# Products with v of the half-density slots placed behind the first share of the next slot

## What is computed

```python
scores = where(causal, -1e9, q @ k.T / 8 + min(-(cum[i] - cum[j]), 0))   # 4 batches x 8 heads, 576 positions, head size 64
x = softmax(scores) @ v                                                  # 2304 tokens x 512
h = maximum(maximum(x @ w1, x @ w2), x @ w3)                             # 512 -> 768
y = h @ w_out                                                            # 768 -> 512
out = ((y @ w_a) * (y @ w_b)) @ w_out2                                   # 512 -> 1536 -> 512
```

## Time and profile before

| | us |
|---|---|
| median of three runs | 954.92 |
| the profiled execution | 955.04 |
| its span, first to last instruction | 953.3 |
| TensorE matmul busy | 912.0 (96%) |
| VectorE busy | 641.0 (67%) |
| ScalarE busy | 482.3 (51%) |
| GpSimd busy | 339.1 (36%) |

### The profile page before, as it was taken

The page is one execution under the profiler, slowest core; times in us unless marked ns, Lnnn a source line. Parts: engine busy times, 40 slices in busy tenths (PEclk is TensorE's granted clock), DMA queues, the critical chain, the costliest instruction groups (busy, mean ns, idle before and its releaser), DMA issues.

```text
span 953.3 us, 16860 instructions
## 1 busy us (share of the span) xinstructions
PE 912.0 (96%) x5992; PEld 895.2 (94%) x5992; DVE 641.0 (67%) x1369; ACT 482.3 (51%) x1071; POOL 339.1 (36%) x453
## 2 busy tenths in 40 slices
PE   3779899999999999999999999999999999999998
PEld 2578899999999999999999999999999999999998
DVE  6889878877766667664226587868577675676750
ACT  4777776676565655644223445443344443444420
POOL 6867555544243342331001423342133422234200
PEclk9999999999999999999999999999999999999999
DMA  3645232222222122200030342222131112111101
GB/s 117 217 154 159 76 110 66 66 67 93 66 63 59 41 88 66 63 9 15 15 122 2 117 138 95 88 68 73 39 134 60 51 50 76 53 58 54 45 1 67
DMA packets 32225, 71.42 MB, mean 75 GB/s; under 512 B 3600, under 2 KB 18032, under 8 KB 32112
## 3 DMA queue, kind: packets, MB, share of 16 engines
q1 hardware_dynamic: 32144, 70.36, 23.3%
HBM read 60.40 MB, written 9.88 MB: 74 GB/s over the span
## 4 chain that ended last, share of the span: by engine, by line
PE 93%; issue 2%; DVE 2%; ACT 1%; POOL 1%; DMA 1%; SPq 0%; POOLq 0%; DVEq 0%; ACTq 0%
PE bank L1417 28%; PE bank L1292 24%; PE bank L1424 16%; PE bank L1312 8%; PE bank L1243 6%; PE bank L1273 6%; PE bank L1259 5%; DVE soft L942 0%; POOL soft L548 0%; DMA qk_st<-cum_row 0%; DMA qk_raw<-in_qk 0%; ACT soft L619 0%; ACT qk_st L610 0%; DMA x_raw<-in_s 0%; POOL qk_st L539 0%
## 5 line engine op out<-in xcount | busy, mean ns | idle before, releaser
L548 POOL TENSOR_SCALAR soft<-soft,rden 128x576 f32<-128x576 f32 (+4 forms) x160 | 102.3, 658 | 215.5 <-DVE rden L928 215.5
L1292 PE MATMUL bank<-xs_hi,w_hi 128*128 128x256 f32 (+1 forms) x576 | 173.7, 302 | 2.5 <-DVE xs_lo L963 1.9
L1292 PE MATMUL bank<-xs_hi,w_lo 128*128 128x256 f32 (+1 forms) x576 | 170.4, 296 | 0.0
L1292 PE MATMUL bank<-xs_lo,w_hi 128*128 128x256 f32 (+1 forms) x576 | 170.3, 296 | 0.0
L942 DVE CUSTOM_DVE_ANT_0 soft<-bank,causal 64x576 f32<-64x576 f32 (+4 forms) x160 | 85.3, 540 | 46.1 <-PE bank L1243 44.7
L619 ACT ACTIVATE soft<-soft,neg_max 64x576 f32<-64x576 f32 (+4 forms) x160 | 96.0, 600 | 36.0 <-DVE neg_max L942 34.8
L1292 PEld LDWEIGHTS bank<-xs_hi,w_hi 128*128 128x128 f32 x576 | 109.1, 189 | 4.0 <-DVE xs_lo L963 2.1
L1292 PEld LDWEIGHTS bank<-xs_lo,w_hi 128*128 128x128 f32 x576 | 109.3, 190 | 1.1
L1292 PEld LDWEIGHTS bank<-xs_hi,w_lo 128*128 128x128 f32 x576 | 109.1, 189 | 0.0
L1243 PE MATMUL bank<-qk_st 128*128 128x256 f32 (+4 forms) x384 | 92.8, 358 | 16.9 <-DMA qk_st<-cum_row 14.0
L951 DVE TENSOR_TENSOR pt_lo<-bank,pt_hi 128x320 fp32r<-128x320 f32 (+4 forms) x160 | 76.0, 488 | 47.3 <-ACT pt_hi L626 45.3
(11 more groups left out here) (127 smaller groups left out, 2188.8 us busy)
## 6 DMA issues: line engine op xcount, KB each, us to landing
qk_raw<-in_qk SPq DMA_DIRECT2D x32, 576.0 KB, 3.9
raw_even<-in_w SPq DMA_DIRECT2D x18, 512.0 KB, 3.6
raw_odd<-in_w SPq DMA_DIRECT2D x17, 512.0 KB, 3.4
w_raw<-in_w SPq DMA_DIRECT2D x16, 384.0 KB, 3.9
v_raw<-in_v SPq DMA_DIRECT2D x32, 160.0 KB, 2.2
y_raw<-y_dram SPq DMA_DIRECT2D x3, 1536.0 KB, 8.3
outT<-o_stage SPq DMA_DIRECT2D x24, 192.0 KB, 1.9
qk_raw<-in_qk SPq DMA_DIRECT2D x8, 256.0 KB, 3.2
```

The lines of the kernel that those rows point to most:

```text
L548: nc.gpsimd.tensor_scalar(part, part, rden[n % 2][:, i:i + 1], 1.0, ALU.mult, ALU.mult).then_inc(prob_done, 1)
L1292: ins = nc.tensor.matmul(up_ps[g][:, 0:width1(c)], up1_w(w, f, g, kc), x[:, kc, 0:width1(c)], start=(kc == 0 and at == 0), stop=(kc == KC ...
```

## The change

The product of job n - 2 moves from the end of slot n - 1 to slot n, behind its first share, for the slots n = 10 to 24. In slot 24 the product of job 23 keeps its place at the end as well, since slot 25 is of the other kind. ScalarE's `other_half` and VectorE's `x_add` of the moved products move too: behind the exponentials of tiles 0 and 1, and behind `h_lo_sub`. All waits stay as they are.

```diff
--- before.py
+++ after.py
@@ -135,6 +135,12 @@
 def sparse(n):
 
     return place(n)[0] is not None and place(n)[0] < DENSE
+
+
+def outputs_of(n):
+
+    after = n - 2 if sparse(n - 1) else None
+    return after, None if sparse(n + 1) else n - 1
 
 
 def tile_count(n):
@@ -691,9 +697,12 @@
                 rows, downs, rest, ahead = rows_of(n), downs_of(n), rest_of(n), ahead_of(n)
                 if pending_row(n) is not None:
                     h_hi_copy(*pending_row(n))
-                other_half(m - 1)
+                if outputs_of(n)[0] is None:
+                    other_half(m - 1)
                 exp(n, 0)
                 exp(n, 1)
+                if outputs_of(n)[0] is not None:
+                    other_half(m - 1)
                 if rest is not None:
                     x_hi(rest, KC - 1)
                 elif rows:
@@ -1047,9 +1056,12 @@
                 rows, rest, ahead = rows_of(n), rest_of(n), ahead_of(n)
                 neg_scores(n, 0)
                 neg_scores(n, 1)
-                x_add(m - 1)
+                if outputs_of(n)[0] is None:
+                    x_add(m - 1)
                 if pending_row(n) is not None:
                     h_lo_sub(*pending_row(n))
+                if outputs_of(n)[0] is not None:
+                    x_add(m - 1)
                 pt_lo_sub(m, 0)
                 neg_scores(n, 2)
                 if rest is not None:
@@ -1360,6 +1372,8 @@
             def sparse_slot(n):
                 m = n - 1
                 share(n, 0)
+                if outputs_of(n)[0] is not None:
+                    output(outputs_of(n)[0])
                 transposes(m, 0)
                 if tile_count(n) > 2:
                     scores(n, 2)
@@ -1377,7 +1391,8 @@
                 if tile_count(m) > 1:
                     transposes(m, tile_count(m) - 1)
                 share(n, 2)
-                output(m)
+                if outputs_of(n)[1] is not None:
+                    output(outputs_of(n)[1])
                 for k in first_scores(n + 1):
                     scores(n + 1, k)
```

## The result

| | before | after |
|---|---|---|
| median, us | 954.91 | 966.65 (966.05 to 966.88, four runs) |
| profiled execution, us | 955.04 | 966.8 |
| its span, us | 953.3 | 965.0 |
| mean granted clock | 1.000 | 0.996 |

The change makes the kernel slower: ratio 1.0119 [1.0106, 1.0132] (in brackets the 95% interval), +11.7 us. The forecast was +6.9 us, and its range ended at 964.5. The direction was right, the time lies outside the range.

What follows compares the result with a forecast made beforehand. TensorE was taken to bound the kernel, with VectorE binding slots 9 to 16. Terms of +0.4 at slot 18, then +2.6, +0.9 and +3.0, made +6.9 us: 961.8 us forecast, range 957.5 to 964.5.

Steps and rivals of the forecast that it cites:

- What bounds the kernel now: Whole kernel: TensorE holds 93% of the chain of waits; VectorE binds slots 9 to 16, where TensorE's wait is VectorE's lateness.
- the wait that goes: Slots 17 to 23: TensorE's stall before the product disappears, 0.74 us each in 18 to 22, 1.35 in 17, 0.37 in 23.
- the wait that comes: Five-tile jobs: transposes(m, 1) shares bank 3 with the product and waits for x_done, 1.85 - 0.59 = 1.26 us.
- Chunk 1, sum: Five-tile slots 18 to 24: +2.6 us over slots 18 to 22, +0.9 in slot 23, +3.0 in slot 24.
- 4 x 0.34 = +1.4 at slot 14: Slots 10 to 13: ScalarE's moved copy delays pt_hi, for which VectorE waits, by 0.34 us a slot.
- more disturbance: VectorE-bound slots: a VectorE subtraction slowed by GpSimd, 0.5 us in each of four slots, giving 963.8; chance 0.06.
- The clock: Slot 15: TensorE's 3.8 us wait halves its clock, share and product take up to twice as long, 963.2; chance 0.07.
- the first of them ends at 131.5, and slot 17 starts at 131.6: End of slot 16: x_lo, 2.2 us late behind the moved sum, bounds slot 17's start, 131.6 instead of 130.50: +1.1.
- Chunk 0 gives back: Slots 9 to 16: VectorE's idle time absorbs the copy and x_lo is on time, 959.3, or down to 957.5; chance 0.13.
- the new wait is hidden: Five-tile slots: transposes(m, 1) finds x_done already set, so only stalls go and the kernel ends near 950.6; chance 0.04.
- Other queues: GpSimd's split_v and SP's loads wait for the moved product or later events, but add nothing to the time.

Runs made afterwards that it cites:

- e1: The changed kernel, with transposes(m, 1) of five-tile jobs writing bank 6 or 7 and the x_done wait moved to transposes(m, 2): 960.69 us, ratio 1.0057.
- e7: The kernel before, TensorE's list untouched, with only other_half and x_add placed as in the change in slots 10 to 16: 958.01 us, ratio 1.0031.
- e4: The changed kernel plus unread matmuls ahead of the first share, 24 in slot 15 and 12 in slot 17: 964.51 us, ratio 1.0096.
- e11: The changed kernel plus 24 unread matmuls ahead of the first share of slot 15 only: 964.58 us, ratio 1.0097.
- e5: The changed kernel with ScalarE's m_copy behind the first pt_hi in slots 10 to 14: 965.75 us, ratio 1.0111.

## Why the prediction was wrong in size

- **"What bounds the kernel now", "the wait that goes", "the wait that comes"**: right. Slots 18 to 23 take 11.78 us (forecast 11.85); from transpose to transpose it is 1.77 us (174.80 to 176.57), where it was 0.47: a stall of 1.30, forecast 1.26, in print 1.10 as forecast. Slot 24 grew by 3.0 us, as forecast. e1 shows it by its absence. "Chunk 1, sum" gave 6.5 us from slot 18 to the end, measured 6.1.
- **Chunk 0, "4 x 0.34 = +1.4 at slot 14"**: the step failed in size. I took the copy at its length less an overlap; without the overlap it costs 0.45 us, and slots 10 to 12 lost 0.57 each in the mean. The rest is VectorE's subtractions, 0.08 a slot in these and 0.28 in slot 13 (1.89 against 1.61), what the rival "more disturbance" (0.06) spoke of, smaller. By slot 14 that is 1.0 us more than forecast. e7 shows that it lies in the two lists; how much of it the place of the copy makes and how much VectorE's subtractions, no run parts cleanly.
- **The clock, "Chance 0.07"**: the step that failed most. The sum put the clock's cost at nothing. The wait came out as worked out (forecast 3.8 us, measured 3.73), and the forecast itself rested on it, so the rival's condition was as likely as the forecast, and only its effect was open. Beside it stood the rows that spoke for the effect and none against it: the waits of up to 1.2 us that I named, and the one of 1.86 at 58.41 that I passed over, left the clock up, but say nothing of 3.8. The chance should have been near one half (an estimate), and the time 963.2 or more. The clock fell twice, for 1.46 and 1.54 us; e4 gives 2.1 us of it back in the medians and 2.9 in the profiles. The Trainium skill, "TensorE: Matmul & The Clock Gate", section "HAM oscillation — how this bites in real kernels", says that long waits bring the half rate back. By that rule the first fall was to be expected, and the trace agrees: 3.73 us without a matmul, then a granted clock of 0.50.
- **Slot 17, "the first of them ends at 131.5, and slot 17 starts at 131.6"**: x_lo was not the bound. With its real place (134.04) the share would have started at about 134.3; it waited for ScalarE's `y_copy`, which stands behind the late x_hi in the same list: 0.7 us more. x_lo itself came as worked out, 9.7 us behind the start of slot 16 (forecast 9.8). I had followed the sum on VectorE and left ScalarE's list out. From slot 17 to slot 18 the forecast was 0.7 less than before; measured are 0.8 more, with a fall of 1.54 in it: right but for the clock.
- **"Chunk 0 gives back"** (0.13) and **"the new wait is hidden"** (0.04) did not come: slots 10 to 13 each lost (0.24 to 0.82 us), and the cover was as short as read. **Other queues**: right, nothing of `split_v` or of SP's loads shows in TensorE's waits; GpSimd's weight subtraction ahead of slot 15 does, as forecast, 0.16 us longer than before (0.88 against 0.72).

Of the 5.0 us missed ahead of slot 18, 1.0 to 1.2 are chunk 0's pace, 0.7 `y_copy`, 3.0 the clock.

## What to carry to other kernels

A product moved away from a wait brings the wait of whatever reuses its bank: count what stands between the last write and the next user of the bank against the whole way through the engines that read it (here 0.59 against 1.85 us), and move the bank too. When a sum forecasts a wait far longer than any in the trace, what TensorE's clock does behind it is part of the sum and not a tail. Where a slot is bound by a side engine, an instruction moved onto that engine's way can cost its full length in each slot (here 0.45 us); taking another off it again gave less, since VectorE's subtractions changed with it.

## What the runs showed of the hardware

Two things I had not expected. The granted clock fell to 0.50 behind a wait of only 1.81 us in the kernel after, and stayed at 1.00 behind a wait of 1.81 us in e11 and one of 1.86 in the kernel before: what decides between them stays open. And VectorE's 64x320 float32 subtraction takes 0.49, 0.77 or 1.13 us in slots that do the same work. In e5 it and the GpSimd subtraction that starts with it take 0.49 and 1.23 us or 1.22 and 0.88, so a slot's length jumps (9.5 or 10.1 us) where one would expect it to glide.
